# Fused attention, MoE and cosine MoE on one core: pairs of heads normalised one period later in the periods without groups, five dummy matmuls a period, weights split over more periods

## The reference, cut to what matters

```python
# attention: batch 4, heads 8, positions 576, width 64; blocks of 64 positions, causal by block
scores = (1 / sqrt(64)) * q @ k.T
scores = where(block_i >= block_j, scores, -1e9)
attn = exp(scores - max(scores)); attn /= sum(attn) + 1e-9
x = heads_side_by_side(attn @ v)                 # (2304, 512)
# MoE: d_ff 768
h = maximum(maximum(x @ w1, x @ w2), x @ w3)
y = h @ w_out                                    # (2304, 512)
# second MoE: d_ff 2048
g = (y @ w_in) * cos(y @ w_in)
out = g @ w_out2
```

## Time and profile before

| | us |
|---|---|
| median of 3 runs | 938.62 |
| lowest and highest | 934.83, 940.88 |
| the profiled execution | 938.85 |
| its span in the trace | 937.1 |
| PE busy in the span | 909.8 |

### The profile page before, as it was taken

One profiled execution on the slowest core, in us unless ns is written; L12 is line 12 of the kernel. 1 busy time (PEld: TensorE's weight loads), 2 busy tenths in 40 slices (PEclk: granted clock), 3 DMA queues, 4 the chain that ended last, 5 costly groups with the idle time before them and its releaser, 6 DMA issues.

```text
span 937.1 us, 15506 instructions
## 1 busy us (share of the span) xinstructions
PE 909.8 (97%) x5632; PEld 847.5 (90%) x5632; DVE 530.3 (57%) x1048; ACT 490.1 (52%) x1016; POOL 235.4 (25%) x232
## 2 busy tenths in 40 slices
PE   7887999999999999999999999999999999999998
PEld 6776889999999999999999999999899998999986
DVE  4677895454653545532111488677576576576564
ACT  3565654343443434442232488666566666566564
POOL 5675543544353553411244000000000000000000
PEclk6977999999999999999999999999999999999999
DMA  5567533223332223210601240100100200200000
GB/s 141 136 156 171 132 64 83 62 61 89 65 83 60 63 77 77 69 35 14 202 23 41 92 148 1 55 14 1 67 0 0 68 0 0 67 0 0 34 1 34
DMA packets 52775, 58.35 MB, mean 62 GB/s; under 512 B 25785, under 2 KB 36313, under 8 KB 52715
## 3 DMA queue, kind: packets, MB, share of 16 engines
q1 hardware_dynamic: 48603, 51.20, 20.4%
q10 hardware_dynamic: 4112, 6.36, 2.3%
HBM read 38.34 MB, written 9.51 MB: 51 GB/s over the span
## 4 chain that ended last, share of the span: by engine, by line
PE 77%; ACT 3%; DVE 3%; issue 1%; POOL 0%; POOLq 0%; ACTq 0%; DVEq 0%
PE M_ps L637 7%; PE M_ps L639 7%; PE M_ps L638 7%; PE S_ps L717 4%; PE S_ps L716 4%; PE S_ps L715 4%; PE O_ps L693 3%; PE O_ps L691 3%; PE O_ps L692 3%; PE M_ps L693 3%; PE M_ps L691 3%; PE M_ps L692 3%; PE M_ps L647 3%; PE M_ps L649 3%; PE M_ps L648 3%; PE O_ps L613 2%
## 5 line engine op out<-in xcount | busy, mean ns | idle before, releaser
L637 PE MATMUL M_ps<-x,w_h 128*128 128x288 f32 x576 | 171.8, 298 | 0.7 <-DVE x L776 0.7
L639 PE MATMUL M_ps<-x,w_h 128*128 128x288 f32 x576 | 170.2, 295 | 0.0
L638 PE MATMUL M_ps<-x,w_l 128*128 128x288 f32 x576 | 170.2, 295 | 0.0
L637 PEld LDWEIGHTS M_ps<-x,w_h 128*128 128x128 f32 x576 | 108.6, 189 | 1.8 <-DVE x L776 0.9
L638 PEld LDWEIGHTS M_ps<-x,w_l 128*128 128x128 f32 x576 | 108.7, 189 | 0.0
L639 PEld LDWEIGHTS M_ps<-x,w_h 128*128 128x128 f32 x576 | 108.6, 189 | 0.0
L1029 ACT ACTIVATE away<-rest 128x384 f32<-128x384 f32 x96 | 50.5, 526 | 98.9 <-DVE rest L856 98.9
L748 DVE TENSOR_REDUCE neg_max<-S_ps 128x1 f32<-128x448 f32 (+4 forms) x160 | 71.0, 482 | 53.4 <-PE S_ps L556 52.9
L949 ACT ACTIVATE pt_h<-T_ps 128x448 fp32r<-128x448 f32 (+1 forms) x98 | 49.5, 505 | 85.3 <-PE T_ps L596 84.5
L1118 POOL TENSOR_TENSOR h_l<-h_f,h_h 128x288 fp32r<-128x288 f32 x48 | 39.2, 816 | 186.8 <-ACT h_h L967 186.8
L787 DVE TENSOR_TENSOR m_tmp<-M_ps,m_tmp 128x288 f32<-128x288 f32 x48 | 21.9, 456 | 98.5 <-PE M_ps L639 98.5
(11 more groups left out here) (118 smaller groups left out, 2386.6 us busy)
## 6 DMA issues: line engine op xcount, KB each, us to landing
qk_hl<-qk_hm SPq DMA_DIRECT2D x64, 144.0 KB, 2.5
qk_raw<-qT SPq DMA_DIRECT2D x32, 144.0 KB, 3.1
qk_raw<-kT SPq DMA_DIRECT2D x32, 144.0 KB, 3.7
w_raw<-w ACTq DMA_DIRECT2D x6, 768.0 KB, 5.0
inv_b<-inv_d SPq DMA_DIRECT2D x16, 288.0 KB, 3.6
y_d<-y_out SPq DMA_DIRECT2D x32, 144.0 KB, 1.8
y_raw<-y_d SPq DMA_DIRECT2D x6, 768.0 KB, 4.5
out<-o_out SPq DMA_DIRECT2D x18, 256.0 KB, 2.1
```

The lines of the kernel that those rows point to most:

```text
L637: mm(o, w_h, x_h, start=k == 0, stop=False)
L638: mm(o, w_l, x_h, start=False, stop=False)
L639: last = mm(o, w_h, x_l, start=False, stop=k == KM - 1)
```

## The change

In the bare periods: the sums of a pair are gathered a period later (`sum` has lag 3 there), and its normalisation too (norm1, norm_high and norm_low lag 5, norm0 lag 6); in all periods the reciprocals are read back a period later (`inv_in` lag 4, was 3). Only the pair that ends with item 7 is read back at lag 3 (`inv_soon`), in period 10. The dummies before x1 go; five `fill` steps of 320 columns stand in the bare list instead, into the bank of x4, each behind a wait for DVE's reading of that bank. In the full periods ACT does `qk_split` in place of POOL. Every list is put in another order, `W_LOADS` begins at period 1 and `W_SPLIT` at period 6.

```diff
--- before.py
+++ after.py
@@ -80,28 +80,33 @@
 
 
 
-LAG = {"x1": 1, "x2": 1, "x3": 1, "x4": 1, "vA": 2, "vB": 2, "vC": 2, "vD": 2, "take": 2, "sum": 2, "inv": 3, "inv_out": 3, "inv_in": 3,
-       "norm0": 5, "norm1": 4, "norm_high": 4, "norm_low": 4, "split": -1, "load": -1, "load_v": 1, "split_v": 1}
+LAG = {"x1": 1, "x2": 1, "x3": 1, "x4": 1, "vA": 2, "vB": 2, "vC": 2, "vD": 2, "take": 2, "sum": 2, "inv": 3, "inv_out": 3,
+       "inv_in": 4, "norm0": 5, "norm1": 4, "norm_high": 4, "norm_low": 4, "split": -1, "load": -1, "load_v": 1, "split_v": 1}
+
+FIRST_LAST = H - 1
+LAG["inv_soon"] = 3
+LAG = {"full": LAG, "bare": dict(LAG, sum=3, norm0=6, norm1=5, norm_high=5, norm_low=5)}
 PE_PERIOD = {
-    "bare": ["s1", "s0", "x1", "x2", "vA", "s4", "x3", "vB", "m", "vC", "vD", "x4"],
-    "full": ["vA", "s1", "vB", "vC", "s0", "x1", "x2", "vD", "G1", "x3", "s4", "G3", "m", "x4", "G2"],
+    "bare": ["s1", "s0", "x1", "x2", "vA", "fill", "s4", "fill", "fill", "vB", "m", "x3", "vC", "fill", "fill",
+             "x4", "vD"],
+    "full": ["vA", "vB", "vC", "s1", "vD", "s0", "x1", "x2", "G1", "x3", "s4", "G3", "x4", "m", "G2"],
 }
 DVE_PERIOD = {
-    "bare": ["s0", "s1", "inv", "s4", "norm0", "x1", "norm1", "x2", "norm_low", "W1", "x3", "x4", "W2"],
-    "full": ["norm0", "norm1", "s0", "inv", "x1", "norm_low", "s1", "G1", "x2", "s4", "G3", "W1", "x3", "x4",
-             "G2", "W2"],
+    "bare": ["s1", "s0", "x1", "s4", "norm0", "norm1", "inv", "W1", "x2", "x3", "norm_low", "W2", "x4"],
+    "full": ["s0", "inv", "norm1", "norm0", "s1", "x1", "norm_low", "G1", "x2", "s4", "G3", "x3", "W1", "G2",
+             "x4", "W2"],
 }
 ACT_PERIOD = {
-    "bare": ["W1", "W2", "load_w", "x1", "x2", "m", "x3", "take", "norm_high", "x4"],
-    "full": ["W1", "load_w", "x1", "norm_high", "x2", "take", "G1", "x3", "G3", "m", "x4", "W2", "G2"],
+    "bare": ["x1", "load_w", "W1", "W2", "x2", "m", "x3", "norm_high", "x4", "take"],
+    "full": ["W1", "x1", "take", "norm_high", "load_w", "x2", "G1", "split", "x3", "G3", "x4", "m", "W2", "G2"],
 }
 POOL_PERIOD = {
     "bare": ["q_low", "k_low", "split", "split_v"],
-    "full": ["q_low", "k_low", "split_v", "G1", "split", "G3", "G2"],
+    "full": ["q_low", "k_low", "split_v", "G1", "G3", "G2"],
 }
 SP_PERIOD = {
-    "bare": ["load", "load_v", "copy_k", "inv_out", "copy_q", "m", "sum", "inv_in"],
-    "full": ["load", "inv_out", "load_v", "copy_q", "copy_k", "m", "G1", "G3", "inv_in", "sum", "G2"],
+    "bare": ["sum", "load", "copy_k", "load_v", "copy_q", "m", "inv_in", "inv_out", "inv_soon"],
+    "full": ["inv_in", "load", "sum", "load_v", "inv_out", "copy_k", "G1", "m", "copy_q", "G3", "G2"],
 }
 
 G_SLOTS = [0] * 11 + [5, 5, 5, 6, 5, 5, 5, 5] + [6, 5, 6, 5, 6, 5, 6, 5] + [6, 5, 6, 5, 5, 5, 5, 5, 5]
@@ -122,9 +127,9 @@
 LOAD_OF = {p: n for n, pieces in enumerate(LOADS) for p in pieces}
 LATER = 16
 
-W_SPLIT = {8: (0,), 9: (1, 2), 10: (3, 4, 5), 11: (6, 7, 8, 9, 10), 12: (11, 12, 13, 14, 15, 16),
-           13: (17, 18, 19, 20, 21, 22, 23)}
-W_LOADS = {2: 0, 4: 1, 6: 2, 8: 3, 9: 4, 10: 5, 11: 6, 12: 7}
+W_SPLIT = {6: (0,), 7: (1,), 8: (2, 3), 9: (4, 5), 10: (6, 7), 11: (8, 9, 10, 11, 12), 12: (13, 14, 15, 16, 17),
+           13: (18, 19, 20, 21, 22, 23)}
+W_LOADS = {1: 0, 3: 1, 5: 2, 7: 3, 8: 4, 9: 5, 11: 6, 12: 7}
 assert len(PIECES) == N_IN + KF2 and len(LOAD_OF) == N_P1
 
 TC = 384
@@ -162,8 +167,6 @@
 WARM = 12
 FILL = 512
 
-FILLS = 2
-
 ZEROED = 5
 
 
@@ -171,7 +174,8 @@
 
     for n in range(N_PERIODS):
         g, pieces = G_FIRST[n], list(dict(weights).get(n, ()))
-        for name in period_steps(names["full" if G_SLOTS[n] else "bare"], G_SLOTS[n], len(pieces)):
+        kind = "full" if G_SLOTS[n] else "bare"
+        for name in period_steps(names[kind], G_SLOTS[n], len(pieces)):
             if name == "G":
                 step("G", g)
                 g += 1
@@ -180,7 +184,7 @@
                 if pieces:
                     step("weights", pieces.pop(0))
                 continue
-            item = n - LAG.get(name, 0)
+            item = n - LAG[kind].get(name, 0)
             if FIRST_ITEM.get(name, 0) <= item < N_MAIN:
                 step(name, item)
 
@@ -464,7 +468,7 @@
                     sum_in(n)
                 elif name == "inv_out" and n % 2:
                     inv_out(n)
-                elif name == "inv_in" and n % 2:
+                elif (name == "inv_in" and n % 2 and n != FIRST_LAST) or (name == "inv_soon" and n == FIRST_LAST):
                     inv_in(n)
                 elif name == "G" and GROUPS[n][1] == "out":
                     store_y(n)
@@ -573,9 +577,6 @@
                     pe.wait_ge(pt_low["2"], n + 1)
                 else:
                     pe.wait_ge(pt_low["3" if s == "1" else "4"], n)
-                if s == "1" and n < ROOMY:
-                    for _ in range(FILLS):
-                        fill(step_bank(n, s))
                 if s == "1":
                     pe.wait_ge(qk_copied[n % 2], 32 * (n // 2 + 1))
                     pe.wait_ge(q_low, n + 1)
@@ -660,6 +661,11 @@
                     turned_scores(n, name[1:])
                 elif name[0] == "v" and name[1:] in VALUES:
                     values(n, name[1:])
+                elif name == "fill":
+
+                    if n >= 2:
+                        pe.wait_ge(pt_low["4"], n - 1)
+                    fill(step_bank(n - 1, "4"))
 
 
             def fill(bank):
@@ -928,9 +934,13 @@
                     act.dma_start(wo_raw[:, k:k + 3, :], w_out[k * P:(k + 3) * P, :].rearrange("(k p) f -> p k f", p=P)
                                  ).then_inc(w_loaded[n], 16)
 
-            def first_split():
-                act.wait_ge(qk_loaded[0], 32)
-                A(qk_hm[0:D, 0, PAD:PAD + 2 * S], qk_raw[0:D, 0, 0:2 * S], ACT.Copy).then_inc(qk_high, 1)
+            def qk_split(n):
+                act.wait_ge(qk_loaded[n % 2], 32 * (n // 2 + 1))
+                if n >= 3:
+                    act.wait_ge(turned["4"], n - 2)
+
+                    act.wait_ge(qk_high, n)
+                A(qk_hm[0:D, n % 3, PAD:PAD + 2 * S], qk_raw[0:D, n % 3, 0:2 * S], ACT.Copy).then_inc(qk_high, 1)
 
             def maxima(n):
                 act.wait_ge(m_turned, n + 1)
@@ -988,6 +998,8 @@
                     exps(n, name[1:])
                 elif name == "m":
                     maxima(n)
+                elif name == "split":
+                    qk_split(n)
                 elif name == "load_w" and n in W_LOADS:
                     load_weights(W_LOADS[n])
                 elif name == "take":
@@ -1010,7 +1022,7 @@
             act.wait_ge(consts_set, 1)
 
             A(scratch, half_pi, ACT.Exp)
-            first_split()
+            qk_split(0)
             walk(step, ACT_PERIOD, W_SPLIT)
             act.wait_ge(x_lowed, N_MAIN // 2)
             for g in range(G_FIRST[N_PERIODS], N_GROUPS):
```

## The result

The changed kernel takes 943.45 us (median of 9 runs, 939.01 to 948.66), the kernel before 938.1 (9 runs, 934.83 to 940.88). The ratio is 1.0066, with a 95% interval of 1.0039 to 1.0092: slower by two thirds of a per cent, where 928.1 us was forecast. The profiled execution took 944.91 us, its span is 943.1.

The account below looks back on a forecast made before the run. It took full periods from 141.28 us as bound by PE's own work, with gains only in the earlier bare and first full periods: 938.85 - 9.9 (periods 3 to 10, to 59.1) - 1.8 + 1.0 = 928.1 us; range 915 to 938.

Parts of the forecast that it names:

- the one on odd periods: Bare odd periods: PE 6.2 us; weight loads ahead of v might delay it, from nothing up to 2 us a pair.
- 13.3, 13.4, 14.5 and 15.1: Forecast us for the bare period pairs (3, 4), (5, 6), (7, 8) and (9, 10), sum 56.3.
- one fall of the clock: Periods 3 to 10: one drop of PE to 1.2 GHz in place of two, at 2.8 us; ends 0 and 7.2.
- DVE's norms and pieces of weights: Bare periods: norms 0.75 us each, pieces 0.68 to 1.9; pair (9, 10), with 4 pieces, put at 15.1 us.
- B: Rival, chance 0.28: DMAs stay the limit, contention moves to v and the maxima; pairs 14.5, two clock falls, 934.5 us.
- The floor of 6.2 a period: Bare periods: PE's own work of 5.44 us plus about 0.8 for five dummies, taken as 6.2 us.
- D: Rival, chance 0.06: DVE and POOL exclude each other, five DVE instructions at their long ends in even periods; 936.7 us.
- C: Rival, chance 0.09: inv_b lands late in odd full periods and PE waits, 1.6 us in each of ten; 950.4 us.
- A: Rival, chance 0.17: bare periods run clean, no clock fall, loads land in 3 us, pairs at 12.5; 915.9 us.
- periods 11 to 13: First three full periods: 43.2 us forecast, 1.8 less than before, with about 2 us of waiting at group 0.
- lost after: Full periods from 14: later norms cost 0.1 us in each of ten odd periods, 1.0 us more.
- The even periods' own length: Bare even periods: 6.2 to 7.7 us, depending on when the load of q and k lands.

Follow-up runs that it names:

- e2: Changed kernel with the first six weight loads cut to a quarter of their bytes, the rest zeros set by DVE at the start; 939.26 us.
- e4: Changed kernel without its five dummies; 943.16 us, ratio 1.006 to the kernel before.
- e1: Changed kernel with the weight loads back in the periods of the kernel before; 940.25 us, ratio 1.0031 to the kernel before.
- e5: Changed kernel with weight loads at a quarter of their bytes and the bare norms moved to odd periods; 945.12 us, ratio 1.0094 to the kernel before.
- e10b: Kernel before with only the changed kernel's W_LOADS, issued behind x1 in ACT's list; 945.24 us, ratio 1.0072 to the kernel before.
- e6: Changed kernel with each of six weight loads cut into four of 192 KB, two or three a period over periods 1 to 10; 936.13 us.

## Why the prediction was wrong

**The failed step** is the one on odd periods: "v landing 4 us later less the slack of some 2 us is 2 us a pair" as the upper end, and of that almost nothing taken, "because the even loads no longer meet a weight load just issued". The pairs took 17.15, 19.49, 18.65 and 21.08 us, against 13.3, 13.4, 14.5 and 15.1: 20.07 more. Less the 2.8 that I had set apart for one fall of the clock, that is the 17.3 us by which the stretch (76.37) misses 59.1. The other terms miss by half a microsecond together, the other way, so the 16.8 us between 944.91 and 928.1 lie in the pairs.

Not all of it is the failed step. The first three pairs hold 14.09 of the 20.07, and each has its wait at x1. The last pair holds 5.98 and has none: its idle places, 2.31, 1.01, 1.00 and 1.74 us, together 6.06, all end on DVE, which is busy there for 18.33 of 21.08 us. So a second term was too small, that of DVE's norms and pieces of weights at their short ends in the pair (9, 10): two of the pieces in these periods took 1.89 and 1.86 us, and two norms 2.36. How much of that is DVE's own is open, since DVE got x1 of period 8 only after 4.64 us of idle time and was behind from there on.

Three things went wrong in the failed step. I priced v alone, by its landing of 6.7 to 8.3 us in period 9, while the maxima and both copies of q and k stand on the same queue within 3.3 us of v. The row of the maxima and the copy of q's low part are the ones with the least slack: issued at 31.67 and 30.39, wanted at 33.93. Then I credited the slack of v to all of them. And I priced the DMAs by their share of 0.66 (in B), where the question was who is issued in the 5 us after 768 KB: in the even periods that grew most, the share was 0.32 and 0.42.

**What makes the 17.3 us** can be read from the windows. PE was idle for 76.37 - 57.82 = 18.55 us; the forecast held 59.1 - 49.6 - 2.8 = 6.7, so 11.85 are idle time that was not forecast. The three waits at x1 are 11.55, and of the other 7.0 nearly all, 6.06, are the waits on DVE in periods 9 and 10. PE's work of 57.82 us is 9.26 above eight periods at 6.07; 2.8 were forecast, 6.46 were not. Some 0.7 of these lie in periods 7 and 10 at full clock (6.31 and 6.56 us), the rest is clock. The floor of 6.2 a period was 0.13 too high, 1.04 in eight. 11.85 + 6.46 - 1.04 = 17.27. That each long wait has a lower clock in its period stands in the rows (0.85, 0.75, 0.85 in periods 4, 6 and 8); PE's work is 1.66, 3.03 and 1.64 us above 6.07 there, so a wait of 3.40, 4.32 and 3.83 us cost 1.4 to 1.7 times its length.

**B**, the rival that had "the contention moves from q and k to v and the maxima", named the mechanism. The sign given for it, an idle place ahead of s1 behind POOL in each even period, did not come; the wait stands at x1, behind the DMAs themselves. Its price, 14.5 a pair, was too low for the same reason, and it was given 0.28. **D** is there in part (e2, and periods 7, 9 and 10 elsewhere): its sign, a mean above 1.2 us, did not come (995 and 997 ns). What it costs the changed kernel was not isolated: the 6.06 us of waits for DVE in periods 9 and 10 are the most that bears its name, with the clock behind them, and the attempts to move the norms brought other waits. **C** did not come: from 146.66 to 425 PE is busy for all 278.34 us. **A** was refuted by the first even period after (11.13, where the sign for the forecast was "period 4 below 7.5 us").

**Right** were: the sums' wait on DVE goes; an odd period is PE alone (6.07, forecast 6.2); periods 0 to 2 do not move; periods 11 to 13 in 43.04 (43.2), with 2.13 us at group 0 (2); 0.6 us lost after (1.0); dummies that cost and gain almost nothing in sum (e4). The even periods' own length was right too, where traffic is small (6.60 and 6.82 in e2, forecast 6.2 to 7.7).

**What stays open**: why e1, with the loads in the periods of before, takes 2.2 us more than the kernel before; its waits for POOL at s1 and for v in period 10 are seen, but the parts of the new order behind them were not separated. What DVE's overrun costs by itself. Why e5 is slower than e2 by its median and not in its trace. And why the DMA engines drain the weight load of period 3 so unevenly.

## What to carry to other kernels

Before a large background transfer is moved, list every transfer issued in the microseconds after it on any queue, with its size and the moment its consumer wants it: the price was set here by those with the least slack, one of 2.5 KB and one of 144 KB, not by the mean DMA share. Cut such a transfer into parts and spread them over the periods before anything is reordered around it: this took 7.3 us off the changed kernel and 3.6 off the old one, while none of the reorderings tried made either kernel faster than the one before. Price a stall of PE with the slow clock that follows it, and test one edit by itself on the old kernel (e10b here) when a change of many parts goes wrong.

## What the runs showed of the hardware

A 2.5 KB transfer, issued 3.2 us after one of 768 KB on another queue, let PE go on only 4.9 us after the end of its issue; one of 144 KB, issued 1.9 us after it, took 6.6 us to landing. For 2 us of that time the 16 DMA engines were busy for only a tenth or two. The Trainium skill ("DMA: Bandwidth & Descriptors", section "Queues, rings and completion order") says that an engine takes turns between its queues packet by packet; by that rule a small transfer would not have to wait for a large one to end. The trace shows it late all the same, in step with v, which was issued ahead of it on its own queue. With the same bytes as transfers of 192 KB, two a period and half a microsecond apart, the waits in the same place were 0.65 us and less in periods 3 to 6 (e6).

With the weights' traffic small, two norms on DVE beside POOL took 3.31 us for 1.5, and one piece of weights 1.89 us, where another took 0.70 (e2). And the slow clock stayed long: after 2.35 us of idle time between 60.9 and 64.9 us in e2, PE ran at 1.2 GHz up to 78 us, although it was busy for all of these 13.1 us.
